# Reordering the entry and the first batch of a three-stage attention kernel, with DMA copies of K and earlier reciprocals

## The reference

```python
# stage 1: 8 heads of 64, causal window of 128 keys, ALiBi bias
scores = q @ k.T / 8 - slope[h] * |rel|          # masked outside 0 <= rel < 128
x = softmax(scores) @ v                          # (4, 576, 512)
# stage 2: gated MLP with a product over tokens
h = relu(x @ w_in); u, v = h[..., :512], h[..., 512:]
v_n = (v - mean(v)) / sqrt(var(v) + 1e-6)
x = (u * (einsum('ts,bsd->btd', w_spatial, v_n) + b_spatial[:, None])) @ w_out
# stage 3: 4 experts, each a causal attention of one head of 64; the 2 best by x @ w_gate
for e in range(4):
    y = softmax(causal((x @ wq[e]) @ (x @ wk[e]).T / 8)) @ (x @ wv[e]) @ wo[e]
    out += weight_of_top2(x @ w_gate)[e] * y
```

## Time and profile before

| | us |
|---|---|
| median of three runs | 610.12 |
| lowest and highest | 610.01, 611.67 |
| profiled execution | 609.56 |
| its span, first to last instruction | 607.8 |

### The profile page before, as it was taken

One profiled execution on the slowest core, in us unless ns is written; L12 is line 12 of the kernel. 1 busy time (PEld: TensorE's weight loads), 2 busy tenths in 40 slices (PEclk: granted clock), 3 DMA queues, 4 the chain that ended last, 5 costly groups with the idle time before them and its releaser, 6 DMA issues.

```text
span 607.8 us, 12100 instructions
## 1 busy us (share of the span) xinstructions
PE 561.7 (92%) x4416; PEld 481.7 (79%) x4416; DVE 368.6 (61%) x1243; ACT 333.4 (55%) x975; POOL 260.4 (43%) x445
## 2 busy tenths in 40 slices
PE   3797989998999989999999999999999999999895
PEld 1576978598877779999787778999787678999784
DVE  4996452257778873246778873236777884336773
ACT  2876432145668683334768773234767864324662
POOL 5765313024525752243534653252633664151521
PEclk9998999999999999999999999999999999999997
DMA  8900821000000033020000015020000000000001
GB/s 233 262 2 23 238 70 55 25 1 1 36 28 18 2 87 71 0 79 2 23 24 36 1 43 116 1 79 0 20 27 36 2 1 1 1 1 2 1 36 44
DMA packets 29743, 26.23 MB, mean 43 GB/s; under 512 B 5810, under 2 KB 22194, under 8 KB 29684
## 3 DMA queue, kind: packets, MB, share of 16 engines
q1 hardware_dynamic: 29684, 25.46, 15.0%
HBM read 20.74 MB, written 4.72 MB: 42 GB/s over the span
## 4 chain that ended last, share of the span: by engine, by line
PE 75%; DVE 11%; POOL 5%; issue 4%; ACT 3%; DMA 1%; SPq 1%; DVEq 0%; POOLq 0%; ACTq 0%
PE bank L1095 16%; PE bank L1097 16%; PE bank L1096 16%; PE bank L1126 9%; PE bank L1085 9%; PE bank L1111 3%; POOL p L513 2%; DVE neg L934 2%; PE bank L1275 2%; DVE pt_lo L842 2%; PE bank L1276 2%; ACT q L672 1%; POOL ring L430 1%; DVE q L997 1%; DMA kz<-kT 1%
## 5 line engine op out<-in xcount | busy, mean ns | idle before, releaser
L1095 PE MATMUL bank<-pt_hi,vv 128*64 128x128 f32 (+1 forms) x528 | 107.5, 235 | 13.0 <-issue 8.0
L842 DVE TENSOR_TENSOR pt_lo<-bank,pt_hi 128x512 fp32r<-128x512 f32 (+5 forms) x176 | 84.2, 493 | 41.7 <-ACT pt_hi L582 40.1
L430 POOL TENSOR_SCALAR ring<-ring,r 128x256 f32<-128x256 f32 (+2 forms) x160 | 73.8, 474 | 78.9 <-DVE r L792 78.9
L1097 PE MATMUL bank<-pt_hi,vv 128*64 128x128 f32 (+1 forms) x528 | 101.4, 224 | 0.0
L1096 PE MATMUL bank<-pt_lo,vv 128*64 128x128 f32 (+1 forms) x528 | 101.3, 224 | 0.0
L582 ACT CAST pt_hi<-bank 128x512 fp32r<-128x512 f32 (+5 forms) x176 | 72.8, 432 | 51.5 <-PE bank L1126 49.8
L1095 PEld LDWEIGHTS bank<-pt_hi,vv 128*64 128x64 f32 x528 | 71.9, 136 | 27.1 <-issue 20.2
L557 ACT ACTIVATE ring<-ring,neg 128x256 f32<-128x256 f32 (+2 forms) x160 | 75.1, 473 | 16.6 <-DVE neg L780 16.2
L1085 PE MATMUL bank<-kz,q 128*128 128x512 f32 (+2 forms) x160 | 73.9, 551 | 9.6 <-DMA kz<-kT 9.6
L513 POOL TENSOR_SCALAR p<-p,r,wgt 128x128 f32<-128x128 f32 (+4 forms) x80 | 51.9, 653 | 69.9 <-DVE r L792 65.3
L1096 PEld LDWEIGHTS bank<-pt_lo,vv 128*64 128x64 f32 x528 | 72.1, 137 | 8.6 <-issue 2.9
(11 more groups left out here) (143 smaller groups left out, 1614.9 us busy)
## 6 DMA issues: line engine op xcount, KB each, us to landing
q<-qT SPq DMA_DIRECT2D x16, 256.0 KB, 4.2
kz<-kT SPq DMA_DIRECT2D x32, 128.0 KB, 4.4
v_raw<-v SPq DMA_DIRECT2D x16, 256.0 KB, 3.6
out<-o_sb SPq DMA_DIRECT2D x16, 256.0 KB, 2.0
w_in_raw<-w_in SPq DMA_DIRECT2D x2, 1024.0 KB, 7.1
w_cat_raw<-wcat SPq DMA_DIRECT2D x1, 1544.0 KB, 7.0
w_spatial_raw<-wsT SPq DMA_DIRECT2D x1, 1152.0 KB, 10.5
w_outT_raw<-woT SPq DMA_DIRECT2D x1, 1024.0 KB, 5.3
```

The source lines that it names most:

```text
L430: last = nc.gpsimd.tensor_scalar(p, p, r1[0:r, i % 2, h:h + 1], 0.0, ALU.mult, ALU.add)
L842: last = nc.vector.tensor_tensor(pt_lo[0:r, g % 2, c0:c1], bank[0:r, 2 + g % 2, c0:c1], pt_hi[0:r, g % 2, c0:c1].bitcast(F32), ALU.subtract)
L1095: nc.tensor.matmul(to, hi_l, hi_r, start=first, stop=False)
L1097: return nc.tensor.matmul(to, lo_l, hi_r, start=False, stop=last)
```

## The change

Five parts.

- **Entry.** q and K of the first two tiles come by pairs of heads, each with a semaphore of its own (`s_pair_in`); the q of tile 0 comes behind them. The zero halves of `kz` are filled for two tiles by VectorE and GpSimd, for the others by ScalarE, which also fills the zero rows of `vv` from a zeroed buffer. TensorE makes six products on that buffer (`WARM`). The first two tiles of v are split by ScalarE and VectorE instead of GpSimd. The bias table is made in two halves.
- **First batch.** GpSimd's tables are built in four parts at groups 5, 8, 9 and 14. The splits of w_in stand at groups 2, 3, 6, 7 and 10, 11, 14, 15, before at 2 to 5 and 9 to 12. All splits of w_spatial stand ahead of the last tile's statistics.
- **Every batch.** v's last tile is split at group 8 instead of 10.
- **Stage 3, K.** The second copies of the second half of k are made by four transfers of SyncE instead of four GpSimd copies.
- **Stage 3, order.** v3 products, scores and the small work of ScalarE and VectorE are written in another order, and reciprocals are taken up to two groups ahead.

Some waits count anew because of it. No product but the six is added and none taken away.

On GpSimd the copies of k that stood ahead of and between the first scalings are gone. On VectorE the reciprocal of group 13 (277, 278) stands ahead of the last maximum and of the addition into o_sb, where it stood behind them, and group 14's has taken its old place. The diff, cut to its core:

```diff
-SPLIT1 = {2: 3, 3: 6, 4: 10}
+SPLIT1 = {2: 3, 3: 6, 4: 8}
 S1_BANKS = (0, 1)
+WARM = 6
+W_IN_AT = {1: (2, 3, 6, 7), 0: (10, 11, 14, 15)}
...
-            for t in range(2):
-                load_qk(0, t)
-                load_v(0, t)
+            for k in range(HP):
+                c = slice(0, 2 * P)
+                sp.dma_start(q1[:, k, P:2 * P], qT[0, :, k, P:2 * P]).then_inc(s_pair_in[k], 16)
+                for odd in range(2):
+                    half = slice(D * odd, D * odd + D)
+                    sp.dma_start(kz[half, 2 * k + odd, c], kT[0, half, k, c]).then_inc(s_pair_in[k], 16)
+                if k % 2:
+                    load_v(0, k // 2)
+            sp.dma_start(q1[:, :, 0:P], qT[0, :, :, 0:P]).then_inc(s_qk_in[0], 16)
             load_w_in(1)
...
+                for i in (4, 5):
+                    a, m = half_and_part(i)
+                    es, c = slice(2 * (m - 2), 2 * (m - 1)), slice(HALF * a, HALF * a + HALF)
+                    sp.wait_ge(s3_qh, 8 * b + i + 1)
+                    sp.dma_start(k3_hi[D:P, es, c].bitcast(F32), k3_hi[0:D, es, c].bitcast(F32)).then_inc(s3_kc, 16)
+                    sp.wait_ge(s3_qk, 8 * b + i + 1)
+                    sp.dma_start(k3_lo[D:P, es, c].bitcast(F32), k3_lo[0:D, es, c].bitcast(F32)).then_inc(s3_kc, 16)
...
-            nc.gpsimd.memset(kz[0:D, 1::2, :], 0.0).then_inc(s_kz, 1)
+            nc.gpsimd.memset(kz[0:D, 1::2, 0:2 * P], 0.0).then_inc(s_kz, 1)
             nc.gpsimd.memset(q1_flat[:, HP * S:], 0.0)
+            nc.gpsimd.memset(neghalf[:], -0.5)
...
-            for t in range(ORDER1[0] + 1):
-                split_v_hi(0, t)
-                split_v_lo(0, t)
...
-                    if first and g == 0:
-                        tables()
+                    if first and g in (5, 8, 9, 14):
+                        tables((5, 8, 9, 14).index(g), g)
...
-                double_k(2, False)
...
-                scale3(0)
-                scale3(1)
-                pool.wait_ge(s3_sd, NG3 * b + 2)
-                double_k(2, True)
-                double_k(3, False)
-                scale3(2)
-                pool.wait_ge(s3_sd, NG3 * b + 3)
-                double_k(3, True)
+                for g in range(3):
...
+            def high_v_first(t):
+                act.wait_ge(s_v_in[t], 16)
+                nc.scalar.copy(vv[:, t, :, 0:D], v_raw[:, t]).then_inc(s_vh0, 1)
+
+            act.wait_ge(s_warm, 1)
+            for odd in range(2):
+                half = slice(D - D * odd, P - D * odd)
+                nc.scalar.copy(kz[half, odd::2, 2 * P:S],
+                               pt_hi[half, 0, 0:S - 2 * P].bitcast(F32).unsqueeze(1).to_broadcast([D, HP, S - 2 * P])
+                               ).then_inc(s_kzr, 1)
+            nc.scalar.copy(vv[LAST:P, NT - 1], pt_hi[LAST:P, 0, 0:2 * D].bitcast(F32).unsqueeze(1).to_broadcast([P - LAST, H, 2 * D])
+                           ).then_inc(s_vz0, 1)
+            exp1(0, 0)
+            exp1(0, 1)
+            high_v_first(0)
+            exp1(0, 2)
+            high_v_first(1)
...
-                    if first and 2 <= g < 2 + KT:
-                        high_w_in(1, g - 2)
-                    if first and 9 <= g < 9 + KT:
-                        high_w_in(0, g - 9)
+                    for half, at in W_IN_AT.items():
+                        if first and g in at:
+                            high_w_in(half, at.index(g))
...
-                exp3(0)
-                exp3(1)
-                high_v3(1)
-                exp3(2)
-                exp3(3)
-                high_v3(2)
+                for w in range(4):
+                    exp3(w)
+                for t in range(2, NT):
+                    high_v3(t)
+                act.wait_ge(s3_ch, 6 * b + 1)
+                nc.scalar.activation(lexp[:], wsel[:], ACT.Exp).then_inc(s3_le, 1)
+                high_qk(4)
+                high_qk(5)
                 exp3(4)
                 exp3(5)
-                high_v3(3)
-                high_v3(4)
-                act.wait_ge(s3_ch, 6 * b + 1)
-                nc.scalar.activation(lexp[:], wsel[:], ACT.Exp).then_inc(s3_le, 1)
-                for i in range(4, 7):
-                    high_qk(i)
+                high_qk(6)
...
-            nc.vector.memset(kz[D:P, 0::2, :], 0.0).then_inc(s_kz, 1)
-            nc.vector.memset(vv[LAST:P, NT - 1].bitcast(F32), 0.0).then_inc(s_vz, 1)
+            nc.vector.memset(pt_hi[:, 0].bitcast(F32), 0.0).then_inc(s_warm, 1)
+            nc.vector.memset(kz[D:P, 0::2, 0:2 * P], 0.0).then_inc(s_kz, 1)
             dve.wait_ge(s_base, 1)
-            for h in range(H):
-                last = nc.vector.tensor_scalar(bias[:, h, :], base[:], 2.0 ** (-8.0 * (h + 1) / H) / SCALE, None, ALU.mult)
-            last.then_inc(s_bt, 1)
-            dve.wait_ge(s_bt, 1)
+
+            def bias_table(part):
+                for h in range(H // 2 * part, H // 2 * (part + 1)):
+                    last = nc.vector.tensor_scalar(bias[:, h, :], base[:], 2.0 ** (-8.0 * (h + 1) / H) / SCALE, None, ALU.mult)
+                last.then_inc(s_bt, 1)
+                dve.wait_ge(s_bt, part + 1)
+
+            def low_v_first(t):
+                dve.wait_ge(s_vh0, t + 1)
+                nc.vector.tensor_tensor(vv[:, t, :, D:2 * D], v_raw[:, t], vv[:, t, :, 0:D].bitcast(F32), ALU.subtract
+                                        ).then_inc(s_vl0, 1)
+
+            bias_table(0)
             bias1(0, 0)
-            for g in range(1, AHEAD1):
-                bias1(0, g)
-                reciprocal1(0, g - 1)
+            bias_table(1)
+            bias1(0, 1)
+            reciprocal1(0, 0)
+            bias1(0, 2)
+            reciprocal1(0, 1)
+            bias1(0, 3)
+            low_v_first(0)
+            reciprocal1(0, 2)
+            low_v_first(1)
...
+                norm_v(NT - 2)
                 if first:
-                    for t in range(NT - 1):
+                    for t in range(NT):
                         low_w_spatial(t)
-                norm_v(NT - 2)
                 stats_v(NT - 1)
                 norm_v(NT - 1)
                 low_vn_last()
-                if first:
-                    low_w_spatial(NT - 1)
...
-                max3(0)
-                max3(1)
                 low_v3(0)
-                max3(2)
-                max3(3)
+                for w in range(4):
+                    max3(w)
                 low_v3(1)
                 reciprocal3(0)
-                low_v3(2)
                 reciprocal3(1)
+                for t in range(2, NT):
+                    low_v3(t)
+                top2_a()
+                top2_b()
+                low_qk(4)
                 max3(4)
                 max3(5)
-                low_v3(3)
-                low_v3(4)
-                top2_a()
+                low_qk(5)
                 reciprocal3(2)
-                top2_b()
-                low_qk(4)
-                low_qk(5)
                 low_qk(6)
-                done = 6
+                done, inverted = 6, 3
                 for g in range(NG3):
-                    early = 2 < g + 1 < NG3 and end_of(G3, g + 1, E) <= done
-                    if early:
-                        reciprocal3(g + 1)
+                    while inverted < min(NG3, g + 3) and end_of(G3, inverted, E) <= done - max(0, inverted - g - 1):
+                        reciprocal3(inverted)
+                        inverted += 1
                     while done < target3(g):
                         max3(done)
                         done += 1
-                    if 2 < g + 1 < NG3 and not early:
-                        reciprocal3(g + 1)
+                    if inverted < min(NG3, g + 2):
+                        reciprocal3(inverted)
+                        inverted += 1
...
-                        pe.wait_ge(s3_kd, 8 * (b + 1))
+                        pe.wait_ge(s3_kc, 64 * (b + 1))
...
+                v3_product(1)
                 for w in range(4):
                     scores3(w)
-                v3_product(1)
-                v3_product(2)
+                for t in range(2, NT):
+                    v3_product(t)
                 scores3(4)
                 scores3(5)
-                v3_product(3)
-                v3_product(4)
                 for i in range(4, 7):
```

97 lines of the change are left out of this document (56 added, 41 removed).

## The result

The changed kernel takes 590.51 us (median of four runs, 590.41 to 590.63), the kernel before on the same chip 610.58 us (610.01 to 611.67). The ratio is 0.9683, with a 95% interval of 0.9663 to 0.9703: 20.1 us won, where 16.3 us were forecast. The profiled execution took 590.41 us, with a span of 588.3 us against 607.8.

A forecast was written before the change was run, and what follows sets the result against it. TensorE, busy 92% of the span, was taken as the bound, so only its idle time could be won. 2.0 + 1.9 + 2.4 + 3.0 + 2.6 + 4.4 = 16.3 us gave 593.8 us, range 588.0 to 600.0.

The forecast's parts named there:

- everything passes: Rival, chance 0.14: the followers taken as next late don't bind, so 5.4 us more are won: 588.4.
- entry, to V(0): Start of batch 0: K in head pairs brings the first values product 2.0 us earlier (0.1 to 3.0).
- groups 0 to 6, to V(4): Batch 0: moved tables and w_in splits shorten waits totalling 3.7 us; half taken, 1.9 us (0.8 to 3.7).
- V(12) and the clock behind it: Batch 0, values product of group 12: 2.1 of its 3.05 us wait go, plus 1.0 us of clock.
- splits of w_in at groups 14, 15: Batch 0: splits moved to groups 14 and 15, where VectorE has hardly a gap, lose 0.7 us.
- end of stage 1, batch 0: With w_spatial's splits ahead of the last tile's statistics, 2.6 us of the spatial product's 2.77 us wait go.
- stage 1, batches 1 to 3: Attention stage: the earlier split of v's last tile removes 1.0 of a 1.20 us TensorE wait in each batch.
- entry bound by arrivals: Rival, chance 0.18: the entry's transfer lag stays 4.9 us and w_in is late for group 2: 597.6.
- Part (a): Expert stage: GpSimd no longer waits for k before its first scaling; 1.0 us of waits go, 0.55 comes through per batch.
- Part (b): Expert stage: group 13's reciprocal is taken earlier; of a 0.96 us wait, 0.55 us is won per batch.
- Part (c): Expert stage: four copies move from GpSimd to SyncE transfers and cost nothing up to a landing of 2.8 us.
- late copies: Rival, chance 0.04: the expert stage's SyncE copies land late, score 8 waits 4.2 us, 20.8 us are lost: 614.6.

The follow-up runs named there:

- tables at 0: The changed kernel with all of GpSimd's tables built at group 0 again instead of at groups 5, 8, 9 and 14; 589.84 us.
- tile 2 first: Kernel of u half at 9, 10, 13, 17 with Q and K of tile 2 loaded ahead of w_in's v half, split at 3, 4, 6, 7; 588.58 us.
- expert stage alone: The kernel before with only the change's parts of stage 3; 599.69 us, ratio 0.9811.
- u half at 9, 10, 13, 17: The changed kernel with the splits of w_in's u half at groups 9, 10, 13, 17 instead of 10, 11, 14, 15; 586.82 us.

## Why the prediction was right, and where not

It was right in the sign, and 590.51 lies in the range of 588.0 to 600.0, 3.3 us below the forecast of 593.8 and at the very edge of the band of 590.5 to 596.5 that was given 0.53, next to "everything passes" (588.4). That the sum came this near is in part luck: one term failed by 5.2 us to the one side, and the others together by 8.4 us to the other:

| term | forecast, us | measured, us |
|---|---|---|
| entry, to V(0) | 2.0 | 3.6 |
| groups 0 to 6, to V(4) | 1.9 | 1.9 |
| V(12) and the clock behind it | 3.1 | 3.4 |
| splits of w_in at groups 14, 15 | -0.7 | -5.9 |
| end of stage 1, batch 0 | 2.6 | 2.5 |
| stage 1, batches 1 to 3 | 3.0 | 4.0 |
| expert stage | 4.4 | 8.7 |
| last product | none | 1.3 |
| sum | 16.3 | 19.5 |

The measured column is of the two profiled spans, 607.8 and 588.3 us. The end of stage 1 is the lead of 6.0 at the spatial product less the 3.0 at 64.09, less 0.5 that the spatial product itself takes longer (15.56 us instead of 15.08, with the wait for vn_lo in it).

**Entry.** The mechanism was right: first score at 4.22 (forecast near 5), the fourth pair's arrival decides, T(0) stands behind it. Three sizes were off. The last K transfers carry half of the old ones' bytes (64 KB against 128 KB), and not a quarter. SyncE's issues of the small transfers take 0.39 to 0.61 us and not 0.64: the last K of pair 3 is the second of the two issues below, near 7.6 us and not 8.4.

```profile
7.09 1.10 SPq L333 DMA_DIRECT2D kz<-kT  x2
```

The lag from there to 10.04 is 2.4 us, where I took 3.0, and T(0) is at 11.00 and not 12.4. From T(0) to V(0) the 3.4 us of the forecast were 3.2. The rival "entry bound by arrivals" is out, though a relative of it came: fifteen transfers stand ahead of w_in instead of eight, K of tile 2 stands behind w_in, and TensorE waits 1.47 us for it at 20.06. It also waits 1.11 us at 12.71 for the q of tile 0, which now comes behind the pairs. I had asked whether w_in is late, and not what is queued behind it.

**Groups 0 to 6.** 1.9 forecast and 1.9 measured, with the wrong reason in part, so this hit is luck. T(4)'s 1.76 us went and K's 1.47 came, so moving the tables gave 0.3 us, which the run with the tables at 0 confirms; V(4)'s wait fell from 1.95 to 0.29. The half that I took off was taken by the wait for K, which I had not seen. The 1.1 us that the split of group 6 was said to pay again were 0.3.

**Group 13 and the clock.** V(12)'s wait fell by 2.0 us (3.05 to 1.09; forecast 2.1), and the clock stayed at 1.00 there, worth 1.5 us (forecast 1.0). The forecast began with v's split, as in batch 1; here the w_in splits were as much of the cause, since with them back at 9 to 12 V(12) waits 2.93 us though v's split stays at 8, and with v's split back at 10 it waits 1.88. The step that failed is "0.7 lost" for groups 14 and 15. I priced the two passes of VectorE by their length, as if they stood in a queue. They stand in a chain that alternates between ScalarE and VectorE and ends in x_lo, and V(16) waits for x_lo: 2.85 us of wait and, in this trace, 3.05 us of clock, which is 0 or 1.5 us in others. The forecast had named that very mechanism for V(12), and asked of V(16) only whether VectorE had a gap.

**Batches 1 to 3.** 1.33 to 1.37 us each, forecast 1.0. The run with the split of v at 10 shows that this one number brings it all: 1.5 us. I had put 1.20 us as the most that could go. A wait costs more than its idle time. In the two last rows of the fence on the run with the tables at 0, the transposes at 57.56 start while the last value product runs to 57.50 + 0.22 = 57.72; in a stream without a wait the next product overlaps the one before by 0.16 us, and behind a wait it does not. So 1.2 us of idle time are 1.36 us. The 1.50 us of that run have another 0.12 us in them, by which V(16) waits longer (0.59 us instead of 0.47).

**Expert stage.** Forecast 1.1 us a batch, measured 2.2. Part (a), the order: 1.48 us in the lead, of which V(0) gives back 0.2 (T(0) to V(0) 2.69 us before, 2.90 now), forecast 0.55. I had put V(0) next, late by half of the gain; it was hardly late. The two waits, 1.04 us, with the overlap of each, 0.16, make 1.36 of the 1.48. Part (b), reciprocals: 0.57, forecast 0.55. Part (c), transfers: they land at 2.5 us, under the 2.8 of their cover, and never make a score wait; that cost nothing, as forecast, but they also brought 0.35 us, which I had put at nothing. Single steps sum to 2.4 - 0.2, and the batch as a whole shows 2.2. The rival "late copies" is out, and its threshold of 2.8 us was only 0.3 away.

**End of stage 1.** Right in size and in what is next late: the spatial product waits 0.31 us inside for vn_lo.

**Last product.** In the kernel before the last products with w_o took 0.63 us each, now 0.39:

```profile
584.13 0.39 PE L1139 MATMUL bank<-w_o_hi,zt 128*128 128x512 f32 x1
```

and in the trace of before:

```profile
602.81 0.63 PE L1097 MATMUL bank<-w_o_hi,zt 128*128 128x512 f32 x1
```

That is the lower level behind the same wait of 1.74 us for zt. It is 1.3 us in this pair of traces, no part of the change touches it, and other variants show it again (the last batch's groups take 40.3 us with the tables at 0 and 39.2 in the run with tile 2 first). This wait of 1.74 us stands in all fourteen traces, and the clock is low at it or behind it in eight of them. I count it as chance.

**What stays open.** Why the same wait is followed by the lower level in some traces and not in others, and for 3.5 us in some and 7 in others, was not settled. It sets how much of the 5.9 us at V(16) a run pays. Nor was it settled how the spread of the variants' runs divides between the clock and the landing of K of tile 2.

## What to carry to other kernels

A piece of work that two engines share, high part here and low part there, must be priced by the chain that it joins and not by its length: with two of the pieces in the three groups ahead of a split that TensorE waits for, batch 0 lost 5.9 us, half of it by the clock; right behind such splits the whole kernel took 3.7 us less. When a stall goes away in one place, look for it with the same size at the next place of the same kind, because a table that moves four pieces can move the stall with them. When loads are reordered, follow each load behind the moved ones to its first user as well.

## What the runs showed of the hardware

- Behind a wait of 2.85 us TensorE ran at a granted clock of 0.51 in the next 4 us and of 0.64 in the 4 us behind them, and that cost 3.05 us. Behind the same wait in other kernels it stayed at 1.00 (two traces) or cost 1.5 us (three). The same wait of 1.95 us at V(4) was followed by 1.00 in the kernel before and by 0.69 in the run of the expert stage alone. Behind the waits of 0.95 to 1.88 us at V(8), V(12) and V(16) it stayed up in all traces, but it fell behind one of 1.02 us at the entry (u half at 9, 10, 13, 17), and in eight of fourteen traces at the 1.74 us of the last products.
- At the start the granted clock is shown as 1.00 while four products take 3.75 us; six products on zeros ahead bring the same products to 2.54 us. The time does not notice.
- Small transfers are issued by SyncE in 0.39 to 0.62 us each. A K half of 64 KB in the entry's crowd landed 2.4 us after its issue, 144 KB from SBUF to SBUF on a quiet queue 2.5 us.
- A load that was issued in the same place started its reader at 19.24 us in one trace and at 21.56 in another (K of tile 2).
- A wait of TensorE costs its idle time and some 0.16 us more, by which products overlap without a wait: 1.20 us of idle were 1.33 to 1.37 us of time, 2.79 us were 2.97.
